# A three-stage attention and feed-forward kernel: new places for the splitting of the next tile's inputs, one copy moved, one loop redrawn

## The reference

```python
# q, k, v: [8, 8, 576, 64]; keys and values are averaged in groups of 8 -> 72 keys
scores = scale * q @ k_p^T; attn = softmax(scores); x = attn @ v_p     # x: [4608, 512]
h = x @ w_in;  g = max(0.01 * h, h);              x = g @ w_out        # layer 1, d_ff 2048
h = x @ w_in2; g = h * clip(h + 3, 0, 6) / 6;     out = g @ w_out2     # layer 2
```

## Time and profile before

| | |
|---|---|
| time, median of 3 runs | 1744.12 us (1742.31 to 1750.9) |
| the profiled execution: its time, its span | 1742.31 us, 1740.5 us |
| TensorE matmuls busy | 1692.8 us, 97% of the span, 10794 instructions |
| VectorE busy | 1037.1 us, 60% |
| ScalarE busy | 641.8 us, 37% |
| GpSimd busy | 552.3 us, 32% |
| mean TensorE clock granted | 0.994 of full speed |
| DMA | 366.85 MB, mean 211 GB/s |

### The profile page before, as it was taken

One profiled execution on the slowest core, in us unless ns is written; L12 is line 12 of the kernel. 1 busy time (PEld: TensorE's weight loads), 2 busy tenths in 40 slices (PEclk: granted clock), 3 DMA queues, 4 the chain that ended last, 5 costly groups with the idle time before them and its releaser, 6 DMA issues. The chain is left out here.

```text
span 1740.5 us, 34022 instructions
## 1 busy us (share of the span) xinstructions
PE 1692.8 (97%) x10794; PEld 1498.1 (86%) x10794; DVE 1037.1 (60%) x1851; ACT 641.8 (37%) x1305; POOL 552.3 (32%) x651
## 2 busy tenths in 40 slices
PE   7999999999999999999999999999999999999999
PEld 6787888888888888888999888989898888889898
DVE  8686767777686776766454654454544444544444
ACT  4554433433343333333232334343333333333332
POOL 6566674424334343322341303030302121121200
PEclk8899999999999999999999999999999999999999
DMA  5765677867677686767878767675757575767662
GB/s 146 229 197 173 209 243 239 262 208 252 206 232 237 202 260 191 244 202 233 283 214 287 257 178 219 176 222 176 219 177 220 176 221 171 223 174 223 173 200 78
DMA packets 218115, 366.85 MB, mean 211 GB/s; under 512 B 22464, under 2 KB 47040, under 8 KB 218048
## 3 DMA queue, kind: packets, MB, share of 16 engines
q1 hardware_dynamic: 218048, 366.04, 67.6%
HBM read 308.28 MB, written 57.67 MB: 210 GB/s over the span
## 5 line engine op out<-in xcount | busy, mean ns | idle before, releaser
L1412 PE MATMUL ps_h<-xs_hi,ring 128*128 128x256 f32 x3808 | 814.5, 282 | 19.8 <-ACT p L1052 5.5
L1412 PEld LDWEIGHTS ps_h<-xs_hi,ring 128*128 128x128 f32 x3808 | 638.6, 188 | 69.3 <-issue 27.6
L1412 PE MATMUL ps_h<-xs_lo,ring 128*128 128x256 f32 x1904 | 532.0, 279 | 0.0
L1412 PEld LDWEIGHTS ps_h<-xs_lo,ring 128*128 128x128 f32 x1904 | 357.9, 188 | 28.2
L949 ACT ACTIVATE g_hi<-gate 128x512 fp32r<-128x512 f32 x288 | 182.0, 632 | 425.9 <-DVE gate L1132 239.9
L1365 PE MATMUL ps_y<-g_hi,wout_hi 128*128 128x512 f32 x576 | 227.3, 395 | 0.3
L1367 PE MATMUL ps_y<-g_hi,wout_lo 128*128 128x512 f32 x576 | 227.1, 394 | 0.0
L1367 PE MATMUL ps_y<-wout_hi,g_lo 128*128 128x512 f32 x576 | 227.0, 394 | 0.0
L1365 PE MATMUL ps_y<-wout_hi,g_hi 128*128 128x512 f32 x576 | 226.1, 393 | 0.0
L1366 PE MATMUL ps_y<-g_lo,wout_hi 128*128 128x512 f32 x576 | 225.0, 391 | 0.0
L1366 PE MATMUL ps_y<-wout_lo,g_hi 128*128 128x512 f32 x576 | 224.8, 390 | 0.0
(11 more groups left out here) (128 smaller groups left out, 2335.4 us busy)
## 6 DMA issues: line engine op xcount, KB each, us to landing
ring<-w_in_split SPq DMA_DIRECT2D x920, 256.0 KB, 2.8
w_in_split<-ring SPq DMA_DIRECT2D x56, 256.0 KB, 3.9
w_in_split<-stage SPq DMA_DIRECT2D x56, 256.0 KB, 4.0
k_raw<-in_kT SPq DMA_DIRECT2D x32, 288.0 KB, 3.7
q_raw<-in_qT SPq DMA_DIRECT2D x32, 288.0 KB, 4.1
v_raw<-in_v SPq DMA_DIRECT2D x32, 288.0 KB
x0T<-x_stage SPq DMA_DIRECT2D x32, 288.0 KB, 3.9
x1T<-y_stage SPq DMA_DIRECT2D x36, 256.0 KB, 3.6
```

Source lines behind the costliest of these rows:

```text
L1412: mm = pe.matmul(banks[BANK_OF[r]], a, b[:, r, c, :], start=r in OPENS and c == 0 and n == 0, stop=c == 1 and n == 2, skip_group_check=True)
```

## The change

It has three parts. The places of `x_hi` and `x_lo` in tiles 1 to 6 move back by up to three. The copy of the first `ps_y` bank on ScalarE moves from the end of step 0 to a place behind the first copy of step 1, in all tiles from 1 on. VectorE's loop becomes whole tiles 2 to 6; before, steps 0 to 6 of tile 2 and step 7 of tile 6 stood outside it.

```diff
-X_HI_AT = (2, 3, 3, 3, 3, 4, 4)
-X_LO_AT = (2, 3, 4, 5, 6, 7, 8)
+X_HI_AT = (2, 4, 4, 5, 5, 6, 7)
+X_LO_AT = (3, 5, 5, 6, 7, 8, 9)
...
                 nc.scalar.activation(p1[:], banks[0], ACT.Copy).then_inc(p1_ready, 1)
+                if i == 1:
+                    copy_y(T - 1, 0)
                 g_hi_of(s - 1, (i - 1) % HF, 0, before if i == 0 else layer)
...
-                    if m == 7 and i == 0:
-                        copy_y(T - 1, 0)
...
-            for i in range(HF - 1):
-                step(2, i, 1, attention=True)
-
-            with dve.Fori(2, ATT_TILES - 1) as T:
-                step(T, HF - 1, 1, attention=True)
-                for i in range(HF - 1):
-                    step(T + 1, i, 1, attention=True)
-            step(ATT_TILES - 1, HF - 1, 1, attention=True)
+            with dve.Fori(2, ATT_TILES) as T:
+                for i in range(HF):
+                    step(T, i, 1, attention=True)
```

## The result

| | before | after |
|---|---|---|
| median (lowest to highest) | 1749.61 us (1742.31 to 1751.94) | 1759.87 us (1754.70 to 1764.43) |
| ratio of times, 95% interval | 1 | 1.0063 (1.0050 to 1.0078) |
| the profiled execution: time, span | 1742.31, 1740.5 us | 1760.43, 1758.6 us |

The changed kernel is slower by some 11 us. The forecast of 1745.5 and the range up to 1751 missed it. The profiled execution of before turned out to be the lowest of all its runs; beside the experiments the kernel's medians were 1747.22 to 1748.93. The sum started at 1744.12, the median of three runs, where twelve give 1749.61. So of the 14.4 us between forecast and result 5.5 lie in where the sum started (3 to 5 by the medians beside the experiments), and the rest in the change.

A forecast was written before the change was run, and what follows sets the result against it. TensorE, busy for 97% of the span, was taken as the bound, so only its waits could pay. Terms -1.4 + 2.5 + 0 + 0.5 - 0.5 + 0.3 = +1.4 on 1744.1 gave 1745.5 us, range 1739.5 to 1751.

The forecast's parts named there:

- part 3, the restart of VectorE's loop: Jump back between the last remainder and `u`: covered by a 0.68 us remainder, so 0; uncovered perhaps 0.3 in each of four.
- The start of the sum: The time of the kernel before, to which the terms were added: 1744.1 us, a median of three runs.
- Part 1, boundaries 2 to 3 up to 4 to 5: Step 0 behind three tile boundaries: `p` waits behind six roundings, `u` 0.84 us later, a loss of 0.84 each, +2.5 together.
- The 0.62 worked out by the lock rule: Tile boundary 3 to 4: VectorE and GpSimd exclude each other, `gate` shorter by some 0.2, loss 0.62 us a boundary.
- my walk: Instruction-by-instruction timing of VectorE, ScalarE and TensorE through the tile boundaries, worked out with durations from the old trace.
- Boundary 1 to 2: Between tiles 1 and 2: `u` 1.4 us earlier and the 2.12 us wait gone; -1.4 us, from -0.5 to -3.0.
- Boundary 6 to 7: Between tiles 6 and 7: only the `p` wait counts, partly given back by an earlier `h`; +0.5 us, 0 to +0.84.
- Part 2, the copy: ScalarE's moved copy is hidden in 17 tiles and shortens a `p` wait in tile 9; -0.5 us, -0.6 to 0.
- The registers of tile 2: Steps 0 to 6 of tile 2 get register instructions ahead of their waits; +0.3 us, from 0 to 0.75.
- (a): Spreading works: `p` is not held up, boundary waits and tile 9 give back time; -5.2 us, 1738.9; chance 0.13.
- (b): Slower: VectorE's two remainders and loop restart in step 0 bring a `u3` wait to five boundaries; +9.6, 1753.7; chance 0.08.
- (c): Nothing visible: `gate` comes early enough that new and old waits cancel; +0, 1744.1 us; chance 0.09.

The follow-up runs named there:

- run 3: The changed kernel with 60 more waiting instructions ahead of VectorE's loop; 1751.97 us, ratio 1.0016 to the kernel before.
- run 5: The kernel before with 80 waiting instructions ahead on VectorE; 1752.89 against 1748.16 us, ratio 1.0033.
- run 4: The changed kernel with 150 waiting instructions ahead on VectorE; 1765.10 us (five runs), ratio 1.0101 to the kernel before.
- run 2: The kernel before with the new places of roundings and remainders alone, loop and copy as before; 1749.51 against 1747.22 us, ratio 1.0015.
- run 6: The kernel before with 40 waiting instructions ahead on VectorE; 1749.02 against 1748.93 us, ratio 1.0001.
- run 8: The kernel before with the copy moved alone; 1747.20 against 1748.16 us, ratio 0.9996.
- run 1: The kernel before with VectorE's loop redrawn alone, places and copy as before; 1753.67 against 1747.22 us, ratio 1.0036.
- run 7: The kernel before with VectorE's loop redrawn and 60 waiting instructions ahead of it; 1752.34 against 1748.16 us, ratio 1.0025.
- run 9: The kernel before with the copy moved and new places for VectorE's remainders only, old roundings and loop; 1744.58 against 1748.16 us, ratio 0.9984.

## Why the prediction was wrong

**The step that failed is part 3, the restart of VectorE's loop**, "A remainder of 0.68 covers it, I think, so 0; uncovered perhaps 0.3 in each of four". I had looked at what the jump stands beside and not at whether it stays a jump of 0.3 us. The redraw took seven steps of program text out from ahead of the loop; the body moved from about instruction 650 to 461, across four blocks instead of three, and the jump came to 3.2 us, where the prediction had 0, or 0.3 uncovered. The remainders cover 1.5 of it (492.3 to 493.79). In tile 4 `u` starts 4.92 us into the tile in after and 2.86 in run 3, 2.06 later, and group 5 starts 8.25 and 6.18 into it, 2.07 later: the delay passes whole. Over the four boundaries behind the jumps (2 to 3 up to 5 to 6) step 0 takes 62.2 us in after and 53.6 in run 3. These 8.6 us are most of the 9.5. The rest I can't place; it is as large as what the steps of two executions differ by elsewhere.

The start of the sum is a second, smaller part of the miss: the range allowed a median to be off by 2 us, and it was off by 5.5. With the right start the range's upper end would still lie below the result.

The two parts of the redraw that I named are not wrong, only small. It did put the jump where VectorE is late. The old boundary of the loop was at the head of step 7, where VectorE idles; there run 5 loses 1.1 to 1.8 us behind each of its three jumps, and the changed kernel 2.1 to 2.2 behind each of its four.

A rule of the Trainium skill speaks of this, and I had not weighed it. "Runtime: NRT & Kernel Launch", section "Instruction fetch mechanics", says that a taken branch to a target outside the window of blocks that the engine holds must wait for a DMA of the target's block. The runs agree, with 3.2 us against 0.3 and with the q14 packets. They differ in the size: the page gives two blocks of 16 KB, 256 instructions; here the packets have 8 KB, and run 4 is read again though it touches only two blocks of 256. No head makes blocks of 256 fit the six positions.

**Part 1, boundaries 2 to 3 up to 4 to 5: right.** I forecast that group 3 would wait for `p`, that `u` would be later by 0.84 and group 5 with it, and took three such boundaries and none at 5 to 6, +2.5 in all. In run 3 group 3 waits for `p`:

```profile
492.15 0.38 PE L1409 MATMUL ps_h<-xs_hi,ring 128*128 128x256 f32 x1 [0.45 <-ACT p L1052]
```

Counted from the start of group 2, it comes 0.61 later than before (forecast 0.89). `u` comes 2.86 into the tile against 2.27 before, 0.59 later, and group 5 0.58 later. Step 0 takes 0.72, 0.58, 0.58 and 0.57 us more at the four boundaries, 2.45 together: the total is met, with each smaller and one more of them. The 0.62 worked out by the lock rule in the Trainium skill ("SBUF — State Buffer", section "SBUF: two separate sides") was nearer than my 0.84, but not by the way that I gave for it, a `gate` shorter by 0.2. In run 3 `gate` still takes 1.24; what is shorter is the remainder of block 0, which holds VectorE 0.96 us (485.22 to 486.18) where my walk had 1.37. Why it is shorter was not tested.

**Boundary 1 to 2: right.** I forecast -1.4. Step 7 of tile 1 with step 0 of tile 2 took 13.63 + 12.81 = 26.44 us before, 10.47 + 14.39 = 24.86 in run 2 and 24.46 in run 3, so -1.6 and -2.0. The old kernel's own two steps vary, though: with old places and old loop runs 6 and 8 took 25.79 and 26.68. The late remainder of block 1 is what comes next, as the walk said. Behind it TensorE waits for ScalarE's `h`, and not for `p`, which the walk had there:

```profile
277.31 0.38 PE L1407 MATMUL ps_h<-xs_hi,ring 128*128 128x256 f32 x1 [1.28 <-DVE xs_lo L1165]
...
282.90 0.35 PE L1407 MATMUL ps_h<-xs_hi,ring 128*128 128x256 f32 x1 [1.12 <-ACT h L1059]
```

**Boundary 6 to 7: right.** Step 7 and step 0 took 10.77 + 10.58 before and 10.47 + 11.26 in run 3, +0.4 (forecast +0.5).

**Part 2, the copy: right in the trace**, -0.5 worked out and 0.5 gained at its place in tile 9; the time of run 8 can't tell it from nothing.

**The registers of tile 2: about right.** The steps of tile 2 inside the loop take 0.1 us and 0.16 us more at steps 2 and 5, and with the old places tile 2 lasts 106.4 and 107.3 us (runs 1 and 7) against 104.1, 104.9 and 105.9 with the old loop (before, runs 6 and 8; 108.2 in run 5). Of that, 0.3 is all that can be laid to the registers.

**The rivals.** (a) fell: `p` is held up. (b) had the sign, and named the restart and a wait for `u`, but at the third `u` and with 0.3 for the restart; that `u3` slips didn't come about without the stop. Its mechanism, put as a boundary with VectorE's two remainders in step 0, is refuted by run 2, which has just that and loses 0.6 a boundary and no `u` wait. (c) fell by the interval of run 2.

**The sum, done again.** Places +2.6, copy -0.7, the reading 9.5, and the redraw without it 0 to 1.7 give 11.4 to 13.1, where the ratio gives 11.0 (8.7 to 13.6). With the 8.6 us counted where the stop acts it is 10.5 to 12.2.

**Open.** Why a jump needs 2.8 to 4.0 us in the four kernels that have the stop is known in part only. The transfer itself is the least of it. In the changed kernel the first packet behind each jump begins 1.35 to 1.50 us after the branch and takes 0.31, and VectorE's next instruction starts 1.8 after the packet began. That last distance is 1.8 us at 13 of the 15 jumps that stop, and 2.0 and 2.1 at the two where the packet itself took 0.64 and 0.95. What differs is when the packet begins: 1.0 to 1.2 us after the branch in run 1, up to 2.2 in run 5. What fills these times isn't known. That the head of the program has 53 instructions is inferred from where the blocks must lie, not read.

## What to carry to other kernels

An edit that only moves a loop's bounds or takes program text from ahead of it can change whether the loop's body stays in the engine's instruction store. Count the blocks that the body touches (here of 128 instructions), put a long jump where the engine idles rather than on the chain that TensorE waits for, and look for "issue" idle behind the jump and for instruction packets inside the loop. A few idle instructions ahead of the loop tell within one run whether the loop's place is the cause, but they cost time of their own at the start, so the cure is a shorter body or another split.

When preparing work must move, move it on the engine that holds up the consumer and leave the other one alone: late remainders helped (run 9), and late roundings beside them took it back (run 2).

## What the runs showed of the hardware that was not expected

- A loop of 313 instructions on VectorE costs 0.3 us or 3.2 us a jump (2.8 to 4.0 over four kernels), depending on where it begins. The change between the two comes with 40 instructions of padding more.
- The instruction traffic of the whole execution separates the cases too: with the stop `q14` has 51 to 55 packets, without it 34 to 36. The last of these groups, after and then run 3:

```profile
q14 instruction: 54, 0.44, 0.1%
```

```profile
q14 instruction: 34, 0.28, 0.1%
```

- Waits for a count already reached are not free where the engine has to start early: 40, 60, 80 and 150 of these instructions at the head of VectorE's program moved its first sum from 3.7 us to 5.0, 7.4, 9.4 and 16.2 us. In the sequencer's record they start 0.09 to 0.10 us apart. With few of them less is seen, since the first 1.4 us lie in the wait for the keys that is there without padding. In run 4 this brings most of the 5 us or more by which it is slower than after: in the profiled executions 6.3 us, of which tile 1 begins 4.4 later.
